# Gate scores transposed in column strips, and a dense stage in groups of 512 tokens

## The reference

```python
scores = scale * np.matmul(q, k.transpose(0, 1, 3, 2))
scores = np.where(masks[None, :, :, :], scores, -1000000000.0)
...
attn = np.exp(scores)
attn = attn / (np.sum(attn, axis=-1, keepdims=True) + 1e-09)
return np.matmul(attn, v).astype(np.float32)
...
skip_score = x @ w_skip
do_compute = skip_score > 0
logits = xc @ w_gate
e_idx = np.argmax(logits, axis=1)
...
h = np.maximum(xc[mask] @ w1[e], 0.0)
y[mask] = gate_w[mask, None] * (h @ w2[e])
out[do_compute] = xc + y
...
h = x @ w_in
g = np.where(pos, h, np.where(neg, 0.0, (h + beta) ** 2 / (4.0 * beta)))
return (g @ w_out).astype(np.float32)
```

## Time and profile before

| | us |
|---|---|
| median of 3 runs (725.94 to 728.72) | 728.31 |
| the profiled execution | 725.36 |
| its span, first to last instruction | 723.4 |
| PE busy | 673.9 (93%) |
| DVE busy | 349.5 (48%) |
| ACT busy | 236.0 (33%) |
| POOL busy | 150.5 (21%) |

### The profile page before, as it was taken

How to read it: one execution, slowest core, us unless ns; L and a number is a source line. 1 busy time by engine, 2 the same in 40 slices (tenths; PEclk the granted TensorE clock), 3 DMA queues, 4 the chain that set the end, 5 groups by cost and what they waited for, 6 DMA issues and landing times.

```text
span 723.4 us, 11913 instructions
## 1 busy us (share of the span) xinstructions
PE 673.9 (93%) x4432; PEld 616.7 (85%) x4432; DVE 349.5 (48%) x687; ACT 236.0 (33%) x725; POOL 150.5 (21%) x163
## 2 busy tenths in 40 slices
PE   8999894089999999989999999999999999999995
PEld 5878694089999999979989999999999899989994
DVE  3877608214112122367556555555655565556552
ACT  4999814013111111123233223322322332232221
POOL 2555504601122222776001000100100010001001
PEclk8999998579999999999999999999999999999998
DMA  8555192496577777232001000100100010001001
GB/s 266 174 193 207 34 348 82 186 335 239 180 259 264 266 270 267 74 104 72 1 1 45 0 1 0 43 0 0 43 0 0 0 43 0 0 0 43 0 0 43
DMA packets 37774, 73.87 MB, mean 102 GB/s; under 512 B 2676, under 2 KB 16149, under 8 KB 37733
## 3 DMA queue, kind: packets, MB, share of 16 engines
q1 hardware_dynamic: 34860, 63.91, 25.8%
q0 software_dynamic: 2880, 9.52, 3.3%
HBM read 63.48 MB, written 9.94 MB: 101 GB/s over the span
## 4 chain that ended last, share of the span: by engine, by line
PE 86%; ACT 7%; POOL 3%; issue 2%; DVE 1%; DMA 1%; DVEq 0%; SPq 0%
PE pair L942 28%; PE pair L955 18%; PE pair L900 10%; PE bank L910 10%; PE bank L955 9%; ACT prob L477 5%; POOL x_sorted L405 3%; PE pair L852 2%; PE bank L809 1%; PE bank L823 1%; PE pair L796 1%; PE bank L884 1%; ACT XT L485 1%; PE pair L773 1%; PE pair L788 1%
## 5 line engine op out<-in xcount | busy, mean ns | idle before, releaser
L556 ACT ACTIVATE cl<-cl,half 128x384 f32<-128x384 f32 x96 | 59.2, 617 | 189.2 <-DVE cl L751 188.1
L466 POOL DMA_INDIRECT out<-rows_out,tok x18 | 17.4, 965 | 361.3 <-DVE rows_out L739 357.6
L759 DVE TENSOR_TENSOR gl<-gr,gh 128x384 fp32r<-128x384 f32 x96 | 56.3, 586 | 70.0 <-ACT gh L565 68.7
L942 PE MATMUL pair<-yl,WIH 128*128 128x384 f32 x384 | 84.4, 340 | 2.1 <-DVE yl L731 2.0
L751 DVE TENSOR_SCALAR cl<-pair 128x384 f32<-128x384 f32 x96 | 53.4, 556 | 66.9 <-PE pair L942 66.7
L942 PE MATMUL pair<-yh,WIH 128*128 128x384 f32 x384 | 84.4, 341 | 0.9 <-ACT yh L534 0.9
L942 PE MATMUL pair<-yh,WIL 128*128 128x384 f32 x384 | 82.4, 335 | 0.0
L942 PEld LDWEIGHTS pair<-yh,WIH 128*128 128x128 f32 x384 | 69.7, 189 | 9.0 <-ACT yh L534 1.2
L565 ACT CAST gh<-gr 128x384 fp32r<-128x384 f32 x96 | 49.3, 514 | 85.2 <-PE bank L955 60.3
L955 PE MATMUL pair<-WOH,gl 128*128 128x512 f32 x192 | 76.1, 397 | 0.0
L955 PE MATMUL pair<-WOL,gh 128*128 128x512 f32 x192 | 75.8, 395 | 0.0
(11 more groups left out here) (117 smaller groups left out, 938.0 us busy)
## 6 DMA issues: line engine op xcount, KB each, us to landing
WE<-w SPq DMA_DIRECT2D x16, 2048.0 KB, 13.1
xrow<-x_sorted SPq DMA_DIRECT2D x6, 781.5 KB, 10.8
raw_in<-win SPq DMA_DIRECT2D x16, 256.0 KB, 9.1
raw_out<-wout SPq DMA_DIRECT2D x16, 256.0 KB, 2.6
v_loc<-vl SPq DMA_DIRECT2D x4, 768.0 KB, 5.0
q_str<-qT SPq DMA_DIRECT2D x4, 576.0 KB, 5.7
k_str<-kT SPq DMA_DIRECT2D x4, 576.0 KB, 6.8
q_loc<-qT SPq DMA_DIRECT2D x3, 576.0 KB, 5.2
```

The source lines that it names most:

```text
L556: act.activation(cl[:, :], cl[:, :], ACT.Square, bias=half[:, :], scale=0.5).then_inc(squared, 1)
L759: dve.tensor_tensor(gl[:, f % 2, :], gr[:, :], gh[:, f % 2, :].bitcast(F32), ALU.subtract).then_inc(g_low, 1)
L942: last = pe.matmul(h2_b[f % 2][:, 0:G], w[:, c, P * f:P * (f + 1)], x[:, c, :], start=(k == 0), stop=(k == 3 * DC - 1))
```

## The change

The names: SORTED, NS and ST take over 384 for the sorted rows; G becomes 512 for the dense stage, with FULL = 4 groups and REST = 256 tokens.

The gate scores are computed transposed: wgs, 32 columns wide now, is the stationary operand, and XT streams. Four blocks of 512 tokens (j) go to output partitions 32 j to 32 j + 31 of one bank, the last 256 tokens as two blocks of 128 to another bank. DVE and ACT copy both to lgT, PE transposes that (five transposes), and DVE copies the scores to lg in two pieces. Two tiles of rows stand ahead of the transposes, 16 behind; ranks come behind tile 7, the exponential behind the copy of tile 4.

The dense stage has four groups of 512 tokens (up of 12 matmuls of 512, down of 4 x 3) and one of 256 (up of 12 of 256, down of 2 x 3). The finished rows are copied into the part of XT that the group no longer needs (rows_of) and stored from there; the last group uses the first group's part and waits for its stores.

```diff
-EARLY = 4
-RANKS_BEHIND = 10
+EXP_AT = 4
+RANKS_BEHIND = 7
...
-G = 384
-NG, GT = N // G, G // P
+SORTED = 384
+NS, ST = N // SORTED, SORTED // P
+G = 512
+FULL, GT = N // G, G // P
+REST = N - FULL * G
 EXTRA = (N - 1) // WIN
-LGW = 96
+LGW = 32
...
-        yh, _, o = at("yh", [P, DC, G], F32R, h_at)
-        yl, _, o = at("yl", [P, DC, G], F32R, o)
+        yl, _, o = at("yl", [P, DC, G], F32R, h_at)
         gh, _, o = at("gh", [P, 2, G], F32R, o)
-        rows_out, _, o = at("rows_out", [P, GT, D], F32, o)
+        yh, _, o = at("yh", [P, DC, G], F32R, o)
...
-        warm, _, _ = at("warm", [P, 512], BF16)
+        warm, _, _ = at("warm", [P, 512], BF16, h_at)
...
+        lgT, _, o = at("lgT", [P, 512 + P], F32, o)
...
+        lgT_b, lgT_rest_b = bank[4], bank[5]
...
-        h2_b, fin_b = bank[6:8], bank[0:3]
+        h2_b, fin_b = bank[6:8], bank[0:4]
...
+
+        def rows_of(g, t):
+
+            return XT[:, t, bass.ds(0 if isinstance(g, int) and g == FULL else G * g, D)]
...
+            for g in range(NS):
+                sp.dma_start(xrow[:, ST * g:ST * (g + 1), :], xs[SORTED * g:SORTED * (g + 1)].rearrange("(t p) c -> p t c", p=P)).then_inc(sorted_in[g], 16)
...
-            for g in range(NG):
-                for t in range(GT):
-                    if t == 1:
-                        pool.wait_ge(fin_act, g + 1)
-                    else:
-                        pool.wait_ge(fin_dve, 2 * g + (1 if t == 0 else 2))
-                    pool.indirect_dma_start(out, bass.IndirectOffsetOnAxis(tok[:, GT * g + t:GT * g + t + 1], 0), rows_out[:, t, :], None).then_inc(out_done, 16)
-            pool.wait_ge(out_done, 16 * NT)
+            for g in range(FULL + 1):
+                for t in range(GT if g < FULL else REST // P):
+                    pool.wait_ge(fin_act if t % 2 else fin_dve, GT // 2 * g + t // 2 + 1)
+                    pool.indirect_dma_start(out, bass.IndirectOffsetOnAxis(tok[:, GT * g + t:GT * g + t + 1], 0), rows_of(g, t), None).then_inc(out_done if g else first_out_done, 16)
+            pool.wait_ge(first_out_done, 16 * GT)
+            pool.wait_ge(out_done, 16 * (NT - GT))
...
+            act.wait_ge(lgT_ready, 2)
+            act.copy(lgT[0:2 * LGW, 512:512 + P], lgT_rest_b[0:2 * LGW, 0:P]).then_inc(lgT_rest, 1)
             for t in range(NT):
                 act.wait_ge(rows_ready, t + 1)
                 act.copy(xrow[:, t, 0:D], row_b[t % 4][:, :]).then_inc(rows_copied, 1)
-                if t == EARLY + 1:
+                if t == EXP_AT:
                     act.wait_ge(dif_ready, 1)
                     act.activation(ex[:, :, :], dif[:, :, :], ACT.Exp).then_inc(exp_ready, 1)
...
-            def highs(g):
+            def highs(g, n=G):
...
-                    act.copy(yh[:, c, :], XT[:, c, bass.ds(G * g, G)]).then_inc(y_high, 1)
+                    act.copy(yh[:, c, 0:n], XT[:, c, bass.ds(G * g, n)]).then_inc(y_high, 1)
...
-            def finish(g):
-                act.wait_ge(fin_tile, GT * g + 2)
-
-                behind(act, out_done, 16 * GT * g)
-                act.copy(rows_out[:, 1, :], fin_b[1][:, :]).then_inc(fin_act, 1)
-
-            def group(g, last):
+            def finish(g, tiles=GT):
+                for t in range(1, tiles, 2):
+                    act.wait_ge(fin_tile, GT * g + t + 1)
+
+                    if isinstance(g, int) and g == FULL:
+                        act.wait_ge(first_out_done, 16 * GT)
+                    act.copy(rows_of(g, t), fin_b[t][:, :]).then_inc(fin_act, 1)
...
+                    if f == FFC - 1 and following:
 
                         act.wait_ge(h2_ready, FFC * (g + 1))
-                        highs(g + 1)
-                    act.wait_ge(clamped, n + 1)
-
-                    act.activation(cl[:, :], cl[:, :], ACT.Square, bias=half[:, :], scale=0.5).then_inc(squared, 1)
-                    act.wait_ge(g_ready, n + 1)
+                        highs(g + 1, following)
+                    act.wait_ge(clamped, k + 1)
+
+                    act.activation(cl[:, 0:n], cl[:, 0:n], ACT.Square, bias=half[:, :], scale=0.5).then_inc(squared, 1)
+                    act.wait_ge(g_ready, k + 1)
 
...
-                    act.copy(gh[:, f % 2, :], gr[:, :]).then_inc(g_high, 1)
-
-            group(0, False)
-            with act.Fori(1, NG - 1) as g:
-                group(g, False)
-            group(NG - 1, True)
-            finish(NG - 1)
+                    act.copy(gh[:, f % 2, 0:n], gr[:, 0:n]).then_inc(g_high, 1)
+
+            group(0, G, G)
+            with act.Fori(1, FULL - 1) as g:
+                group(g, G, G)
+            group(FULL - 1, G, REST)
+            group(FULL, REST, 0)
+            finish(FULL, REST // P)
...
-            dve.wait_ge(logits_ready, NT)
-            link(dve.tensor_copy(lg[:, :, :], logit_b[:, 0:NE9].rearrange("p (t e) -> p t e", t=NT)))
+            dve.wait_ge(lgT_ready, 1)
+            dve.tensor_copy(lgT[:, 0:512], lgT_b[:, :]).then_inc(lgT_main, 1)
+            dve.wait_ge(logits_ready, 2)
+            dve.tensor_copy(lg[:, 0:16, :].rearrange("p (j q) e -> p q j e", q=4), logit_b[:, :].rearrange("p (q j e) -> p q j e", q=4, j=4)[:, :, :, 0:E + 1]).then_inc(lg_main, 1)
+            dve.wait_ge(lg_main, 1)
+            link(dve.tensor_copy(lg[:, 16:NT, :], gate_b[:, 0:2 * LGW].rearrange("p (j e) -> p j e", j=2)[:, :, 0:E + 1]))
             link(dve.tensor_reduce(top8[:, :], lg[:, :, 0:E], AX_X, ALU.max))
             link(dve.tensor_tensor(dif[:, :, :], lg[:, :, 0:E], tiles(top8[:, :]), ALU.subtract))
...
-            link(dve.tensor_copy(tot[:, :, :], logit_b[:, NE9:2 * NE9].rearrange("p (t e) -> p e t", t=NT)))
+            link(dve.tensor_copy(tot[:, :, :], logit_b[:, 0:NE9].rearrange("p (t e) -> p e t", t=NT)))
...
-            def lows(g):
+            def lows(g, n=G):
                 for c in range(DC):
                     dve.wait_ge(y_high, DC * g + c + 1)
-                    dve.tensor_tensor(yl[:, c, :], XT[:, c, bass.ds(G * g, G)], yh[:, c, :].bitcast(F32), ALU.subtract).then_inc(y_low, 1)
+                    dve.tensor_tensor(yl[:, c, 0:n], XT[:, c, bass.ds(G * g, n)], yh[:, c, 0:n].bitcast(F32), ALU.subtract).then_inc(y_low, 1)
 
...
-            for t in range(NT):
-                if t < EARLY:
-                    rows(t)
-
+            def logits(out, width, first, groups):
                 for c in range(DC):
-                    last = pe.matmul(logit_b[:, (E + 1) * t:(E + 1) * t + LGW], XT[:, c, P * t:P * (t + 1)], wgs[:, c, :], start=(c == 0), stop=(c == DC - 1))
-                last.then_inc(logits_ready, 1)
-            for t in range(EARLY, NT):
+                    for j in range(groups):
+                        last = pe.matmul(out[LGW * j:LGW * (j + 1), 0:width], wgs[:, c, :], XT[:, c, first + width * j:first + width * (j + 1)], start=(c == 0), stop=(c == DC - 1), skip_group_check=True)
+                last.then_inc(lgT_ready, 1)
+
+            logits(lgT_b, 512, 0, 4)
+            logits(lgT_rest_b, P, 2048, 2)
+            for t in range(2):
+                rows(t)
+            pe.wait_ge(lgT_main, 1)
+            for q in range(4):
+                last = pe.transpose(logit_b[:, P * q:P * (q + 1)], lgT[:, P * q:P * (q + 1)], ident)
+            last.then_inc(logits_ready, 1)
+            pe.wait_ge(lgT_rest, 1)
+            pe.transpose(gate_b[:, 0:2 * LGW], lgT[0:2 * LGW, 512:512 + P], ident[0:2 * LGW, 0:2 * LGW]).then_inc(logits_ready, 1)
+            for t in range(2, NT):
                 rows(t)
                 if t == RANKS_BEHIND:
 
                     pe.wait_ge(oh_ready, 1)
                     flat = oh[:, :, :].rearrange("p t e -> p (t e)")
                     pe.matmul(gate_b[:, 0:NE9], before, flat, start=True, stop=True).then_inc(ranks_ready, 1)
-                    pe.matmul(logit_b[:, NE9:2 * NE9], con[:, C_ONE:C_ONE + P], flat, start=True, stop=True).then_inc(ranks_ready, 1)
+                    pe.matmul(logit_b[:, 0:NE9], con[:, C_ONE:C_ONE + P], flat, start=True, stop=True).then_inc(ranks_ready, 1)
...
-            def up(g, f):
+            def up(g, f, tokens):
...
-                        last = pe.matmul(h2_b[f % 2][:, 0:G], w[:, c, P * f:P * (f + 1)], x[:, c, :], start=(k == 0), stop=(k == 3 * DC - 1))
+                        last = pe.matmul(h2_b[f % 2][:, 0:tokens], w[:, c, P * f:P * (f + 1)], x[:, c, 0:tokens], start=(k == 0), stop=(k == 3 * DC - 1))
...
-            def down(g, f):
+            def down(g, f, tokens):
                 if f == 0:
-                    behind(pe, fin_dve, 2 * g)
-                    behind(pe, fin_act, g)
+                    behind(pe, fin_dve, GT // 2 * g)
+                    behind(pe, fin_act, GT // 2 * g)
...
-                for t in range(GT):
+                for t in range(tokens // P):
...
-            def group(g):
-                up(g, 0)
+            def group(g, tokens):
+                up(g, 0, tokens)
                 if not (isinstance(g, int) and g == 0):
```

(21 more changed lines are left out.)

73 lines of the change are left out of this document (37 added, 36 removed).

## The result

| | median us | runs | ratio to before, 95% |
|---|---|---|---|
| before | 728.72 | 5 (725.94 to 731.21) | |
| after | 709.34 | 5 (705.62 to 711.36) | 0.9734 [0.9703, 0.9766] |

The change gains 19.4 us; 13.3 were forecast (715.0, range 711.5 to 721). The profiled execution of after took 705.62 us, span 703.8, so 19.6 us less than the span of 723.4 before.

What follows compares the result with a forecast made beforehand. PE was taken to bound the kernel (busy 93% of the span). Terms -11.6 - 2.0 + 0.8 - 0.6 = -13.4 gave 712.0 for the profiled execution, 714.9 for the median, forecast 715, range 711.5 to 721.

Steps and rivals of the forecast that it cites:

- Gate scores, -11.6: Gate scores before routing: four strips run together, 8 rounds of 0.43 us, scores and everything after 11.6 us sooner.
- a fall of the clock at 91.8: During the gate scores: clock falls to half at about 91.8, back at about 95.2, as in the old profile.
- all behind it: After the scatter: PE's return at 147.33 and all later work move as much as the scores, 11.6 us.
- Two at a time: Gate scores rival, 17%: only two strips' records overlap, 7.3 us for them, 3.9 us lost, total 718.8.
- the rival of no overlap: Gate scores rival, 6%: strips run one after another, scores take 15.6 us, total 726.1, no change that can be told.
- The steps, -2.0: Dense stage steps: 402.2 us before, 354.8 + 45.4 = 400.2 after, so 2.0 less; bounds 4.7 less to 8.6 more.
- 256 columns at 0.121: Dense stage, last group: each 256-column up matmul costs 0.121 us, bounds 0.107 and 0.176.
- the slower rival: Last dense group rival, 4%: 256-column matmuls cost 0.45 us at full float32 price, 63 us more, total 778.
- Cover at the boundaries: Dense group boundaries: PE's cover grows to 8.3 us against a DVE chain of about 7.2, so nothing waits.
- the tail: Kernel end: the last stores finish 2.5 us behind PE instead of 3.14, so 0.6 us less.
- The start of the stage, +0.8: Dense stage start: wider low parts on DVE cost 0.8 us more, bounds 0.4 and 2.5; clock 1.7 us either way.
- The scatter: Rival at POOL's 18 scatters, 7%: they start every 1.91 us instead of 1.40, 9 us come back, total 724.

Runs made afterwards that it cites:

- after_again: The changed kernel measured once more, unaltered, beside the filler versions: 706.74 us, ratio to before 0.9728.
- both_384: Changed kernel with full-group up matmuls cut to 384 columns (first two steps whole) and down matmuls to 384: 625.66 us, one execution, work left out.
- up_384: Changed kernel with only the full groups' up matmuls cut to 384 columns (first two steps whole), downs at 512: 672.38 us, one execution, work left out.
- down_384: Changed kernel with only the down matmuls cut to 384 of 512 columns, full-group ups at 512: 664.82 us, one execution, work left out.
- hold_all: Changed kernel with `hold`'s two dense-start edits, plus 31 useless matmuls in PE's wait for the scattered rows: 706.44 us, ratio to before 0.9704.
- hold: Changed kernel with the first dense up's products reordered and ten useless matmuls between its waits on the low parts: 707.20 us, ratio to before 0.9711.

## Why the prediction was wrong in size

- **Gate scores, -11.6: right in mechanism, -12.55 measured.** The forecast took four strips in rounds of 0.43 us and a fall of the clock at 91.8. The first held: 8 x 0.43 + 8 x 0.11 = 4.3, and 4.50 was measured at full clock. The second did not occur in this execution. In `after_again` it did (0.50 from 90.5 to 93.9, shown above): there from the start of the scores at 90.51 to the first scatter at 105.43 it took 14.92 us, and the forecast had 105.9 - 90.95 = 14.95. Without the fall it is 104.33 - 91.09 = 13.24. So the clock is worth 1.7 us, an item that the forecast took as given from one execution; PE was back 13.3 us sooner and not 11.6. Of this 0.8 was lost again in the wait between the two windows, a term that the forecast did not have: it took "all behind it" to move with 147.33. What stays is 0.9. (The 0.7 us at full clock in the forecast is 0.85 by its own 90.95 and 91.8, which moves its end by under 0.1.) No row showed four strips; the runs do: four column strips took 3.42 us for 32 records where one strip at a time would need 32 x 0.43 = 13.8, four times the rate.
- **Two at a time: refuted**, for the order as written. The other loop order gives about that rate, but not for the rival's reason: there whole strips wait in line, not second records. With four strips side by side the rival of no overlap is out too.
- **The steps, -2.0: this is the step that failed; -8.2 measured.** The term that was mis-sized is "64 x 24 x 0.231 = 354.8". Each matmul took 0.2267, so 348.2: 6.6 us, more than the whole miss of 6.2. The price 0.231 was read from nine downs of 512 columns right behind twelve ups of 384, and carried into a loop where no width changes. There it does not hold, as `both_384` against `up_384` and `down_384` shows. The trace of before had the right price too: at a group boundary two downs follow each other, and the second, shown above at 376.51, has six in 1.36 us, 0.227. The forecast called what goes away "the fixed part of 192 matmuls"; that part is 192 x 0.013 = 2.5 us, and the larger one was the disturbance in 96 mixed steps, 401.5 - 96 x 4.12 = 6.0 us, of which the 16 mixed steps of the last group give some 0.4 back. The total before was put 0.7 us too high (402.2).
- **256 columns at 0.121: right**, 2.87 / 24 = 0.120; the slower rival is refuted.
- **Cover at the boundaries: right**, no wait; so is the tail (2.5 us behind PE).
- **The start of the stage, +0.8: too little, +1.6.** The stretch of waits is 0.6 us longer, but 0.4 of this is its seven wider matmuls (7 x 0.053), which the steps count already. The low clock behind it cost 3.0 and not 1.7 us, so 1.3 more; "absent or twice as long" was in the range, and it came out nearly twice as long. In `after_again`, the same kernel, it lasted 3.4 us and cost 1.7 as before, and the whole start was 1.1 us shorter, 0.5 more than before. `hold_all` shows that it can be absent.
- **The scatter: refuted** as a place where the gain is given back; 23.8 us as before.

Sum of the misses: 0.9 + 6.2 - 0.8 - 0.1 = 6.2 = 19.6 - 13.4. The lower end of the range failed since it took the price of the 512-column matmul as certain, and bounded only the 256-column one.

## What to carry to other kernels

Take the price of an instruction from a stretch in which its neighbours are those that it will have (0.2267 us among its like here, 0.231 in the mixed loop); where a change makes a mixed loop uniform, look for the same instruction among its like in the old trace, even if it stands there only once. The narrow scores gained from column strips issued in turn (4.50 us) and not strip after strip (10.5), so that order is the one to try first for another narrow output. A clock that fell in the one profiled execution is a term with two values (here 13.24 and 14.92 us from the scores to the first scatter), and goes into the range on either side.

## What the runs showed that was not expected

- Four float32 matmuls in four column strips of 32 run at four times the rate of one: 32 records of 512 columns in 3.42 us, eight rounds of 0.43. Issued strip by strip they run mostly two at a time (10.5 us for all 48 records against 4.50), with records from later in the program starting ahead of earlier ones.
- Back to back at a granted clock of 1.00, float32r matmuls start every 0.1733 us at 384 columns, 0.2267 at 512 and 0.120 at 256: 0.417 ns a column and 0.013 us beside them. In the first six to nine matmuls after a change between 384 and 512 (the kernel before, `up_384`, `down_384`) they are slower by 0.02 to 0.04 us in all, in either direction.
- In `hold_all`, with matmuls that fill the waits and the products in another order, the granted clock stayed at 1.00 at the dense start (294 to 324), where it fell to 0.50 in the changed kernel (301.20 to 307.20); in `hold`, with the same two edits there, it fell to 0.50 all the same (303 to 306). At the sort of `hold_all` it fell to 0.50 at 138.5, about 2 us after the last filler had ended, while PE still waited.
